# The chunk loop written out 27 times, or 6 times with a hardware loop of 7 trips between

## The chip, the cores and the metric

The kernel runs on one core of one Trainium2 chip. A NeuronCore has five engines that run their own instruction streams side by side and meet only at semaphores: TensorE (PE, matrix products), VectorE (DVE), ScalarE (ACT), GpSimd (POOL) and SyncE (SP, which here only issues transfers). The metric is the device time of one execution in microseconds (us), the median over several executions.

## The reference, cut to what matters

Three stages follow each other over 12480 tokens of 128 channels: an attention of 49 agents on the keys and of the queries on the agents, and then two two-layer networks of 2048 hidden units.

```
a2k = softmax(scale * agents @ k.T)            # 49 x 12480
agent_v = a2k @ v                              # 49 x 128
x = softmax(scale * q @ agents.T) @ agent_v    # 12480 x 128
h = x @ w_in                                   # 12480 x 2048
g = where(h >= 1, h, where(h <= -1, 0, (h + 1)**2 / 4))
x = g @ w_out                                  # 12480 x 128
r = maximum(x @ w_in2, 0)
out = (s * r*r + b) @ w_out2                   # 12480 x 128
```

## The kernel before, in words

The program is written engine by engine. Each engine has its list of instructions, and the order in it is the order of the source code; there is no scheduler. An instruction names the semaphore count that it waits for and the semaphore that it raises.

After a start-up part of some 55 us (keys and values, the agents' softmax, splitting the weights into a high and a low part in `fp32r` so that two or three products replace one in full precision), the tokens go through in 25 chunks of 500 (`W = 500`, the last chunk 480). A chunk has 16 *items* (`TILES = 16`), one for each block of 128 hidden units. For an item PE does 11 matmuls over 500 columns: 2 for the first network's hidden layer (`ps_h`, lines 559 and 560), 3 for the second network's hidden layer (`ps_h`, lines 578 to 580), 3 that add up the first network's output in `ps_y` (lines 541 to 543) and 3 that add up the second's in `ps_o` (lines 609 to 611). Between them the other engines work on the items: DVE makes `below` (L869), ACT squares it (L672), DVE adds it to `ps_h` (L882), ACT rounds the result to `g_hi` (L680), DVE forms the rest `g_lo` (L864), and PE may then use both for `ps_y`, two items later (`LAG1 = 2`). For the second network ACT takes the positive part (L701) and squares it (L710), and POOL splits it (L1015, L1016, L1018) for `ps_o`, again two items later. The second network is one chunk and four items behind the first. When a chunk's `ps_y` is complete, DVE copies it to `y` (L903, in item 1 of the next chunk), and only then may PE begin the next sum in the same bank (L541, in item 2).

These steps stand in a function `iteration(turns, phase)` of each engine. `all_iterations` calls it for i = 0 to 26, 25 chunks and two more in which the later steps of the last chunks are finished. The buffers form rings of 3 chunks, so the addresses in iteration i depend only on i mod 3 (`CHUNKS_PER_TRIP = 3`). Every semaphore count depends on i itself: item n waits, for instance, for `g1_split` to be at least n + 1. The helper functions accept i as a Python number or as a value in a register of the engine.

```
def at_least(eng, semaphore, count):
    if not isinstance(count, int) or count > 0:
        eng.wait_ge(semaphore, count)

i = turns * CHUNKS_PER_TRIP + phase
for j in range(TILES):
    n, place, there = item(i, phase, j, 0)
```

Before the change i is always a Python number, and the whole program is straight-line: 16412 instructions stand in the trace, 10314 of them PE's weight loads and matmuls.

Of the kernel before, what the change touches and what calls it, by code (L numbers as in the profile page):

```python
# [19 lines left out]
CHUNKS_PER_TRIP = 3  # L20
# [38 lines left out]
def build_program(nc, q, k, v, v_last, agents, w_in1, w_out1, w_in2, w_out2, s_b, out):  # L59
# [5 lines left out]
    CHUNKS = n_queries // W  # L65
# [5 lines left out]
    ITERATIONS = LAST_MLP2 // TILES + 1  # L71
# [4 lines left out]
    BLOCKS = KV_BLOCKS + 1  # L76
    KV_COLS = KV_TILES * 128

    assert C == 128 and n_queries == CHUNKS * W and n_agents < LOW
    assert n_tokens == KV_BLOCKS * KV_COLS + LAST_TILES * LAST_TOK  # L80
    assert MOD % H1_BANKS == 0 and MOD % H2_BANKS == 0 and MOD % SPLIT_RING == 0
# [2 lines left out]
    with ExitStack() as ctx:  # L84
# [232 lines left out]
                eng.wait_ge(semaphore, count)  # L317

        def all_iterations(eng, iteration):
            for i in range(ITERATIONS):  # L320
                iteration(*divmod(i, CHUNKS_PER_TRIP))


# [47 lines left out]
        def _(sp):  # L371
# [25 lines left out]
            def iteration(turns, phase):  # L397
# [7 lines left out]
                if there:  # L405
                    sp.wait_ge(out_ready, c + 1)
                    columns = width(c * TILES)
                    sp.dma_start(out[:, bass.ds(c * W, columns)], out_ring[:, slot, 0:columns]).then_inc(out_slot_free[slot], 16)

            all_iterations(sp, iteration)  # L410

            for slot in range(IO_RING):
# [4 lines left out]
        def _(pe):  # L417
# [128 lines left out]
            def iteration(turns, phase):  # L546
                i = turns * CHUNKS_PER_TRIP + phase
                for j in range(TILES):
# [49 lines left out]
                    if there:  # L598
# [13 lines left out]
                        mm.then_inc(g2_used, 1)  # L612

            all_iterations(pe, iteration)


        @block.scalar
        def _(act):
# [63 lines left out]
            def iteration(turns, phase):  # L682
                i = turns * CHUNKS_PER_TRIP + phase
                for j in range(TILES):
# [35 lines left out]
                    if j == MLP2_DELAY + LAG2 - 1 and chunk(i, phase, -2)[2]:  # L720
# [5 lines left out]
                        nc.scalar.activation(out_ring[:, slot, 0:columns], o_ps[:, 0:columns], ACT.Identity, bias=bias_col[:]).then_inc(out_ready, 1)  # L726

            all_iterations(act, iteration)


# [337 lines left out]
```

## Time and profile before

| | us |
|---|---|
| median of 3 runs | 1107.23 (1107.03 to 1107.34) |
| the profiled execution | 1107.03 |
| its span, first to last instruction | 1105.2 |
| PE busy in the span | 1091.7 |
| ACT / DVE / POOL busy | 923.7 / 915.3 / 841.6 |
| instruction packets fetched | 41 of 0.67 MB in all, 46 of 0.38 MB in all |

The time outside the span is 1107.03 - 1105.2 = 1.8 us. A row of the profile names an engine, a line of the code, the operation, `out<-in`, and its count. Matmuls overlap: a row's duration (0.39 us for 500 columns) is longer than the distance to the next one (0.23 us), and PE is counted busy as long as one of them runs. The queues called "instruction" are the transfers that bring the program itself from memory to the engines.

### The profile page before, as it was taken

What the parts mean: (1) busy time and instruction counts of PE and PEld (TensorE: products, weight loads), DVE (VectorE), ACT (ScalarE), POOL (GpSimd) and SP (SyncE); (2) the same over time, 40 slices, a digit from 0 to 9 for tenths busy, and PEclk for the clock granted to TensorE, in tenths of its full rate; (3) what the DMA queues carried; (4) which work ended last, traced back from release to release, by engine and by line L of the source; (5) the groups of instructions that cost most, each with busy time, mean ns of one, the idle gap of its engine ahead of it and who ended that gap; (6) DMA issues with size and microseconds to landing.
All of it is one profiled execution on the core that took longest, in us unless ns stands there. A gap on an engine that the chain in (4) does not pass through costs nothing.

```text
span 1105.2 us, 16412 instructions
## 1 busy us (share of the span) xinstructions
PE 1091.7 (99%) x5157; PEld 915.8 (83%) x5157; DVE 915.3 (83%) x1456; ACT 923.7 (84%) x1745; POOL 841.6 (76%) x1231
## 2 busy tenths in 40 slices
PE   9999999999999999999999999999999999999998
PEld 8867888888888888888888888888888888888886
DVE  4777888889888888888889888888888888888876
ACT  3276888888888888888888888888888888888887
POOL 3555888788788788788788788788788788788760
PEclk9998999999999999999999999999999999999999
DMA  9700000000000000000000000000000000000000
GB/s 367 287 1 1 1 19 20 1 20 19 1 20 19 1 19 20 1 20 19 1 19 20 1 20 19 1 19 19 3 18 19 10 11 19 13 7 10 10 1 19
DMA packets 11863, 30.84 MB, mean 28 GB/s; under 512 B 1568, under 2 KB 8192, under 8 KB 11264
## 3 DMA queue, kind: packets, MB, share of 16 engines
q1 hardware_dynamic: 11776, 29.79, 7.6%
q8 instruction: 41, 0.67, 0.3%
q14 instruction: 46, 0.38, 0.1%
HBM read 23.40 MB, written 6.39 MB: 27 GB/s over the span
## 4 chain that ended last, share of the span: by engine, by line
PE 97%; DVE 1%; ACT 1%; issue 0%; DMA 0%; SPq 0%; ACTq 0%; DVEq 0%
PE ps_y L541 8%; PE ps_h L559 8%; PE ps_h L578 8%; PE ps_h L580 8%; PE ps_o L609 8%; PE ps_h L579 8%; PE ps_h L560 8%; PE ps_y L542 8%; PE ps_o L610 8%; PE ps_y L543 8%; PE ps_o L611 8%; PE ps_h L446 2%; PE ps_job L424 2%; PE ps_o L472 1%; PE ps_y L472 1%; PE ps_job L432 1%
## 5 line engine op out<-in xcount | busy, mean ns | idle before, releaser
L1018 POOL TENSOR_TENSOR sb_g_lo<-sb_square,sb_g_hi 128x500 fp32r<-128x500 f32 x380 | 484.0, 1274 | 31.7
L882 DVE SCALAR_TENSOR_TENSOR ps_h<-sb_square,ps_h 128x500 f32<-128x500 f32 (+1 forms) x400 | 271.9, 680 | 119.4 <-ACT sb_square L672 118.4
L680 ACT ACTIVATE sb_g_hi<-ps_h 128x500 fp32r<-128x500 f32 (+1 forms) x400 | 235.1, 588 | 101.0 <-DVE ps_h L882 101.0
L864 DVE SCALAR_TENSOR_TENSOR sb_g_lo<-ps_h,sb_g_hi 128x500 fp32r<-128x500 f32 (+1 forms) x400 | 270.6, 677 | 20.2 <-ACT sb_g_hi L680 11.4
L869 DVE TENSOR_SCALAR sb_below<-ps_h 128x500 f32<-128x500 f32 (+1 forms) x380 | 256.7, 675 | 11.2 <-PE ps_h L560 9.9
L701 ACT ACTIVATE sb_relu<-ps_h 128x500 f32<-128x500 f32 (+1 forms) x400 | 235.3, 588 | 24.6 <-PE ps_h L580 11.3
L710 ACT ACTIVATE sb_square<-sb_relu 128x500 f32<-128x500 f32 (+1 forms) x400 | 245.6, 614 | 0.6
L672 ACT ACTIVATE sb_square<-sb_below 128x500 f32<-128x500 f32 (+1 forms) x380 | 233.7, 615 | 0.0
L1016 POOL TENSOR_SCALAR sb_g_hi<-sb_square 128x500 fp32r<-128x500 f32 x380 | 228.3, 601 | 0.0
L1015 POOL TENSOR_TENSOR sb_gate<-sb_ones 1x1 f32<-1x1 f32 x380 | 69.8, 184 | 152.2 <-ACT sb_square L710 150.8
L541 PE MATMUL ps_y<-sb_g_hi,sb_w_out_hi 128*128 128x500 f32 (+1 forms) x400 | 160.7, 402 | 1.2 <-DVE sb_g_lo L864 1.2
L559 PE MATMUL ps_h<-sb_probs_t,sb_m_hi 113*128 113x500 f32 (+1 forms) x400 | 159.3, 398 | 2.4 <-DVE sb_g_lo L864 2.2
L609 PE MATMUL ps_o<-sb_g_hi,sb_w_out_hi 128*128 128x500 f32 (+1 forms) x400 | 155.9, 390 | 1.4 <-DVE sb_g_lo L922 0.9
L578 PE MATMUL ps_h<-sb_y_hi,sb_w_in_hi 128*128 128x500 f32 (+1 forms) x400 | 156.0, 390 | 0.2 <-DVE sb_y_lo L908 0.2
L560 PE MATMUL ps_h<-sb_probs_t,sb_m_lo 113*128 113x500 f32 (+1 forms) x400 | 156.0, 390 | 0.0
L580 PE MATMUL ps_h<-sb_y_hi,sb_w_in_lo 128*128 128x500 f32 (+1 forms) x400 | 155.9, 390 | 0.0
L542 PE MATMUL ps_y<-sb_g_hi,sb_w_out_lo 128*128 128x500 f32 (+1 forms) x400 | 155.6, 389 | 0.0
L543 PE MATMUL ps_y<-sb_g_lo,sb_w_out_hi 128*128 128x500 f32 (+1 forms) x400 | 155.2, 388 | 0.0
L611 PE MATMUL ps_o<-sb_g_lo,sb_w_out_hi 128*128 128x500 f32 (+1 forms) x400 | 155.0, 387 | 0.0
L610 PE MATMUL ps_o<-sb_g_hi,sb_w_out_lo 128*128 128x500 f32 (+1 forms) x400 | 155.0, 387 | 0.0
L579 PE MATMUL ps_h<-sb_y_lo,sb_w_in_hi 128*128 128x500 f32 (+1 forms) x400 | 154.9, 387 | 0.0
L559 PEld LDWEIGHTS ps_h<-sb_probs_t,sb_m_hi 113*128 113x128 f32 x400 | 75.7, 189 | 19.7 <-DVE sb_g_lo L864 3.1
(109 smaller groups left out, 1266.7 us busy)
## 6 DMA issues: line engine op xcount, KB each, us to landing
sb_q_ring<-in_q SPq DMA_DIRECT2D x25, 250.0 KB, 2.8
sb_kv_ring<-in_k SPq DMA_DIRECT2D x12, 512.0 KB, 9.1
sb_kv_ring<-in_v SPq DMA_DIRECT2D x12, 512.0 KB, 15.7
out<-sb_out_ring SPq DMA_DIRECT2D x24, 250.0 KB, 2.1
sb_w_stage<-in_moe_w_out SPq DMA_DIRECT2D x2, 1024.0 KB, 11.7
sb_w_stage<-in_moe_w_in SPq DMA_DIRECT2D x1, 1024.0 KB, 17.8
sb_w_in<-in_moe_w_in SPq DMA_DIRECT2D x1, 1024.0 KB, 17.7
out<-sb_out_ring SPq DMA_DIRECT2D x1, 240.0 KB, 2.0
```

Of the source, the lines that this page charges most:

```text
L541: pe.matmul(y_ps[:, 0:width(n)], hi, g1_hi[:, slot, 0:width(n)], start=(f == 0), stop=False)
L542: pe.matmul(y_ps[:, 0:width(n)], lo, g1_hi[:, slot, 0:width(n)], start=False, stop=False)
L559: pe.matmul(h, m_hi[:, j * 128:(j + 1) * 128], probs_t[:, phase, 0:width(n)], start=True, stop=False)
L560: pe.matmul(h, m_lo[:, j * 128:(j + 1) * 128], probs_t[:, phase, 0:width(n)], start=False, stop=True).then_inc(h1_ready, 1)
L578: pe.matmul(h, hi, y_hi[:, y_slot, 0:width(n)], start=True, stop=False)
L580: pe.matmul(h, lo, y_hi[:, y_slot, 0:width(n)], start=False, stop=True).then_inc(h2_ready, 1)
L609: pe.matmul(o_ps[:, 0:width(n)], hi, g2_hi[:, slot, 0:width(n)], start=(f == 0), stop=False)
L710: nc.scalar.activation(square2[:, place2 % WORK_RING, 0:width(n2)], relu2[:, place2 % WORK_RING, 0:width(n2)], ACT.Square).then_inc(square ...
L864: nc.vector.scalar_tensor_tensor(g1_lo[:, slot, 0:columns], h1_bank(n, place), 0.0, as_f32(g1_hi[:, slot, 0:columns]), ALU.max, ALU.subtra ...
L869: nc.vector.tensor_scalar(below[:, place % WORK_RING, 0:width(n)], h1_bank(n, place), 1.0, 1.0, ALU.min, ALU.subtract).then_inc(below_read ...
L882: nc.vector.scalar_tensor_tensor(h, square1[:, place % WORK_RING, 0:width(n)], 1.0, h, ALU.min, ALU.add).then_inc(g1_summed, 1)
L1018: nc.gpsimd.tensor_tensor(g2_lo[:, place % SPLIT_RING, 0:columns], square, as_f32(hi), ALU.subtract).then_inc(g2_split, 1)
```

## The change

The 27 calls of `iteration` become 3 calls, a loop with `eng.Fori(0, TRIPS)` whose body holds 3 calls, and 3 calls behind it. With `CHUNKS = 25` it is `FIRST_FULL = 3`, `TRIPS = (25 - 1 - 3) // 3 = 7` and `END_FULL = 24`. So iterations 3 to 23 run in 7 trips, and each engine jumps back 6 times. In the loop `trip` is a register of the engine, so `turns`, `i` and all semaphore counts, and the token offset of the query load and of the output store, are computed by the engine itself.

```
-            for i in range(ITERATIONS):
+            for i in range(FIRST_FULL):
+                iteration(*divmod(i, CHUNKS_PER_TRIP))
+            with eng.Fori(0, TRIPS) as trip:
+                for n in range(CHUNKS_PER_TRIP):
+                    turns, phase = divmod(FIRST_FULL + n, CHUNKS_PER_TRIP)
+                    iteration(trip + turns, phase)
+            for i in range(END_FULL, ITERATIONS):
                 iteration(*divmod(i, CHUNKS_PER_TRIP))
```

The loop body of the built program, by engine (an instruction takes 64 bytes: 1.05 MB of fetched packets for 16412 instructions; on PE each of the 564 matmuls of a trip counts twice, with its weight load):

| engine | instructions in the body | KB | register operations in it |
|---|---|---|---|
| PE | 1239 | 79 | 98 + 6 |
| ACT | 408 | 26 | 119 + 5 |
| POOL | 257 | 16 | 62 + 3 |
| DVE | 227 | 15 | 56 + 1 |
| SP | 15 | 1 | 1 + 7 |

The first place is PE where the loop is entered, the first matmuls of iteration 3. In the names, `ps_h_0` is a bank of PSUM, and the names in brackets are the semaphores waited for. Before:

```order
L609 MATMUL ps_o<-sb_g_hi,sb_w_out_hi 128x500 [waits g2_split]
L610 MATMUL ps_o<-sb_g_hi,sb_w_out_lo 128x500
L611 MATMUL ps_o<-sb_g_lo,sb_w_out_hi 128x500
L559 MATMUL ps_h_0<-sb_probs_t,sb_m_hi 128x500 [waits g1_split,probs_t_ready]
L560 MATMUL ps_h_0<-sb_probs_t,sb_m_lo 128x500
L578 MATMUL ps_h_0<-sb_y_hi,sb_w_in_hi 128x500 [waits relu2_ready]
L579 MATMUL ps_h_0<-sb_y_lo,sb_w_in_hi 128x500
L580 MATMUL ps_h_0<-sb_y_hi,sb_w_in_lo 128x500
```

And the same place after the change, where line numbers are 9 higher:

```order
L618 MATMUL ps_o<-sb_g_hi,sb_w_out_hi 128x500 [waits g2_split]
L619 MATMUL ps_o<-sb_g_hi,sb_w_out_lo 128x500
L620 MATMUL ps_o<-sb_g_lo,sb_w_out_hi 128x500
L325 UNCONDITIONAL_BRANCH
L325 ISA
L320 ISA [waits probs_t_ready]
L568 MATMUL ps_h_0<-sb_probs_t,sb_m_hi 128x500 [waits g1_split]
L569 MATMUL ps_h_0<-sb_probs_t,sb_m_lo 128x500
L320 REGISTER_ALU
L587 MATMUL ps_h_0<-sb_y_hi,sb_w_in_hi 128x500 [waits relu2_ready]
L588 MATMUL ps_h_0<-sb_y_lo,sb_w_in_hi 128x500
L589 MATMUL ps_h_0<-sb_y_hi,sb_w_in_lo 128x500
```

The matmuls keep their order; register instructions (`REGISTER_ALU`, and `ISA`, several of them in one) stand between them, and some of these carry a wait that a matmul carried before.

The second place is the same one on ACT. Before:

```order
L672 ACTIVATE sb_square<-sb_below 128x500 [waits below_ready]
L710 ACTIVATE sb_square<-sb_relu 128x500 [waits g2_split,relu2_ready]
L680 ACTIVATE sb_g_hi<-ps_h_2 128x500 [waits g1_used,g1_summed]
L701 ACTIVATE sb_relu<-ps_h_0 128x500 [waits h2_ready]
L672 ACTIVATE sb_square<-sb_below 128x500 [waits below_ready]
L710 ACTIVATE sb_square<-sb_relu 128x500 [waits g2_split,relu2_ready]
```

After:

```order
L681 ACTIVATE sb_square<-sb_below 128x500 [waits below_ready]
L719 ACTIVATE sb_square<-sb_relu 128x500 [waits g2_split,relu2_ready]
L325 UNCONDITIONAL_BRANCH
L325 ISA
L320 REGISTER_ALU [waits g1_summed]
L689 ACTIVATE sb_g_hi<-ps_h_2 128x500 [waits g1_used]
L709 REGISTER_ALU
L710 ACTIVATE sb_relu<-ps_h_0 128x500 [waits h2_ready]
L679 REGISTER_ALU
L681 ACTIVATE sb_square<-sb_below 128x500 [waits below_ready]
```

Here up to three register operations come in for each item, and in 12 of the 48 items of a trip the wait for `g1_summed` stands on a register operation just ahead of the rounding.

The third place is the loop's end on ACT after the change, which the program before does not have:

```order
L681 ACTIVATE sb_square<-sb_below 128x500 [waits below_ready]
L719 ACTIVATE sb_square<-sb_relu 128x500 [waits g2_split,relu2_ready]
L325 REGISTER_ALU
L325 COMPARE_AND_BRANCH
L689 ACTIVATE sb_g_hi<-ps_h_2 128x500 [waits g1_used,g1_summed]
```

The branch follows the last square directly. If it is taken, what runs next is the `ISA` row at the start of the loop, some 400 instructions back.

## Rows read from the trace of the kernel before

**Rows 1.** The page: the span, the engines' busy time, the chain that ended last.

```profile
span 1105.2 us, 16412 instructions
...
PE 1091.7 (99%) x5157; PEld 915.8 (83%) x5157; DVE 915.3 (83%) x1456; ACT 923.7 (84%) x1745; POOL 841.6 (76%) x1231
...
PE 97%; DVE 1%; ACT 1%; issue 0%; DMA 0%; SPq 0%; ACTq 0%; DVEq 0%
```

**Rows 2.** Busy time by stretch (us, counts): the second and sixth trip's stretches.

```profile
289.60:413.10 123.50, 123.50 (x565) 103.41 (x565) 105.46 (x166) 108.31 (x205) 100.61 (x151) 1.00 0.04 13
...
783.50:907.00 123.50, 123.50 (x566) 103.39 (x565) 105.46 (x166) 108.29 (x205) 100.63 (x151) 1.00 0.05 14
```

**Rows 3.** Timeline of PE around 289.65: start, duration, operation.

```profile
288.97 0.39 PE L609 MATMUL ps_o<-sb_g_hi,sb_w_out_hi 128*128 128x500 f32 x1
...
289.65 0.39 PE L559 MATMUL ps_h<-sb_probs_t,sb_m_hi 113*128 113x500 f32 x1
...
293.74 0.39 PE L543 MATMUL ps_y<-sb_g_lo,sb_w_out_hi 128*128 128x500 f32 x1
...
295.78 0.38 PE L541 MATMUL ps_y<-sb_g_hi,sb_w_out_hi 128*128 128x500 f32 x1
```

**Rows 4.** Timeline of PE, the score matmuls of one chunk.

```profile
298.25 0.98 PE L424 MATMUL ps_job<-sb_agents_t,sb_q_ring 128*126 128x49 f32 x8
```

**Rows 5.** Who waited for whom, 289.6 to 413.1: total us, times, longest us.

```profile
POOL sb_gate L1015 <- ACT sb_square L710: 18.7, 39, 1.2
DVE ps_h L882 <- ACT sb_square L672: 15.3, 37, 0.6
ACT sb_g_hi L680 <- DVE ps_h L882: 12.6, 36, 1.1
```

**Rows 6.** DMA queues of the page: packets, MB, share of 16 engines' span.

```profile
q8 instruction: 41, 0.67, 0.3%
q14 instruction: 46, 0.38, 0.1%
```

**Rows 7.** DMA issues: KB each, median us to landing.

```profile
sb_q_ring<-in_q SPq DMA_DIRECT2D x25, 250.0 KB, 2.8
...
sb_agents_t<-in_agents SPq DMA_DIRECT2D x1, 24.5 KB, 1.8
```

**Rows 8.** Timeline of ACT around 289.65.

```profile
287.83 0.59 ACT L680 ACTIVATE sb_g_hi<-ps_h 128x500 fp32r<-128x500 f32 x1 [0.24 <-DVE ps_h L882]
288.48 0.59 ACT L701 ACTIVATE sb_relu<-ps_h 128x500 f32<-128x500 f32 x1
288.96 0.61 ACT L672 ACTIVATE sb_square<-sb_below 128x500 f32<-128x500 f32 x1
289.48 0.61 ACT L710 ACTIVATE sb_square<-sb_relu 128x500 f32<-128x500 f32 x1
290.33 0.59 ACT L680 ACTIVATE sb_g_hi<-ps_h 128x500 fp32r<-128x500 f32 x1 [0.24 <-DVE ps_h L882]
```

**Rows 9.** Timeline of DVE, the copy of a finished `ps_y`.

```profile
293.45 0.68 DVE L864 SCALAR_TENSOR_TENSOR sb_g_lo<-ps_h,sb_g_hi 128x500 fp32r<-128x500 f32 x1
294.17 0.68 DVE L903 COPY sb_y<-ps_y 128x500 f32<-128x500 f32 x1
```

**Rows 10.** Groups by line, 166.19 to 1030.45: shapes, count, busy us, mean ns.

```profile
L541 PEld LDWEIGHTS ps_y<-sb_g_hi,sb_w_out_hi 128*128 128x128 f32 x336 | 63.4, 189 | 10.9
```

**Rows 11.** Timeline of POOL, the split that frees L609 at 288.97.

```profile
286.02 1.29 POOL L1018 TENSOR_TENSOR sb_g_lo<-sb_square,sb_g_hi 128x500 fp32r<-128x500 f32 x1
```

**Rows 12.** Timeline of PE before 70 us, three rows with idle time ahead.

```profile
54.64 1.12 PE L510 MATMUL ps_h<-sb_w_in,sb_agent_v_t 128*113 128x128 f32 x4 [1.43 <-DVE sb_agent_v_t L850]
...
63.02 1.08 PE L424 MATMUL ps_job<-sb_agents_t,sb_q_ring 128*126 128x49 f32 x8 [0.95 <-DVE sb_m_lo L854]
...
69.22 0.49 PE L541 MATMUL ps_y<-sb_g_hi,sb_w_out_hi 128*128 128x500 f32 x1 [1.01 <-DVE sb_g_lo L864]
```

**Rows 13.** Busy time by stretch around them; the third last number is the clock.

```profile
50.00:55.70 5.70, 4.27 (x33) 3.53 (x32) 1.79 (x8) 0.27 (x1) 0.00 (x0) 1.00 0.00 1
55.70:59.10 3.40, 3.27 (x7) 1.92 (x7) 0.59 (x2) 1.46 (x3) 1.02 (x1) 0.50 0.00 0
...
62.00:67.00 5.00, 4.05 (x22) 3.28 (x22) 4.97 (x11) 3.14 (x6) 2.64 (x3) 1.00 0.00 0
67.00:72.00 5.00, 3.99 (x19) 3.09 (x19) 4.12 (x10) 4.66 (x9) 3.58 (x4) 1.00 0.02 5
```

More of the change, by code:

```diff
@@ L77, in build_program @@
     KV_COLS = KV_TILES * 128
+    FIRST_FULL = 3
+    TRIPS = (CHUNKS - 1 - FIRST_FULL) // CHUNKS_PER_TRIP
+    END_FULL = FIRST_FULL + TRIPS * CHUNKS_PER_TRIP
     assert C == 128 and n_queries == CHUNKS * W and n_agents < LOW
```

## The prediction, written before the changed kernel ran

> **What bounds the kernel now.** I read the page's busy line and chain first [rows 1]: PE is busy 1091.7 of 1105.2 us, and 97% of the chain that ended last is PE. The stretches of one trip's length come next [rows 2]: PE is busy 123.50 of 123.50 us, at a granted clock of 1.00, and ACT, DVE and POOL 108, 105 and 101. The 11 matmuls of an item follow each other at some 0.23 us, so an item takes 2.5 us, and nothing in these stretches ends a wait of PE. The waits of the others [rows 5] are ACT, DVE and POOL waiting for each other in PE's shadow. The change leaves every matmul and its order alone. So it can only gain where PE idles, and in the looped part PE never does: a gain is excluded there to within the measurement. It costs what it makes PE idle, and nothing else.
>
> **Part 1, register operations, steady state.** On PE they are 104 in 48 items, two an item. The trace has no such row. The nearest is the row of score matmuls [rows 4]: 8 matmuls and their 8 weight loads in 0.98 us, so PE's sequencer hands out an instruction in 0.06 us or less. An item's 22 then take 1.35 us and 2 more 0.12, of 2.5. I cost them at nothing; the cover is PE's array. From above, an operation as long as a whole hop between ACT and POOL, 18.7 / 48 = 0.39 us an item [rows 5], would come to 1.35 + 0.78 = 2.1, still under 2.5; below nothing it can't be, since it adds work. On ACT, DVE and POOL the operations stand mostly behind an instruction that is running (0.6 us or more), and none of them is on the path. In 12 of 48 items on ACT one stands in the hop from DVE's sum to ACT's rounding, where ACT idles 0.24 us [rows 8]. That hop belongs to a circle (square, sum, rounding, positive part, next square) which is only about 0.15 us short of PE's item time: L701 starts 0.65 after L680 at 287.83, and ACT can start one activation 0.50 after another, as 288.48, 288.96 and 289.48 show. One operation of up to 0.1 us fits in. SP's loads are issued a chunk (41 us) ahead of their use and land in 2.8 us [rows 7]. Cost: 0.
>
> **Part 2, the six jumps back.** The program is fetched in packets [rows 6]: 0.67 MB / 41 = 16 KB on PE's queue, 0.38 / 46 = 8 KB on the other's. 5157 matmuls with their weight loads are 10314 instructions of 64 bytes, 660 KB, in 41 such packets: each is fetched once, as the straight-line program reaches it. At the jump the loop's first packet may be gone. PE's body is 79 KB, 5 to 6 packets, ACT's 26 KB, 4 to 5, POOL's and DVE's 2 to 3. If it is gone, the engine stops for one fetch. No row shows one. From below: the smallest transfer lands in 1.8 us [rows 7], plus the packet's own time, 0.1% of 16 x 1105.2 us / 46 = 0.4 us for 8 KB: 2.2. With PE's packet, 0.3% of the same / 41 = 1.3 us: 3.1. From above: 2.8 + 1.3 = 4.1, the load of 250 KB with it. And zero, if the packet is still there. For ACT I take 2.7, midway between 2.2 and 3.1, as the 1.8 us is for a transfer issued with its addresses at hand.
>
> **What of it is hidden.** I take ACT, as its body is the longest of those with the small packets. Its sequencer gets to the branch when the last square has been let go, not before L701 has ended at 288.48 + 0.59 = 289.07 and not after 289.48, when that square starts [rows 8]. The next trip's first rounding starts at 290.33. That covers 1.26 to 0.85 us. What is late then passes along: the rounding's lateness shrinks by the 0.15 us of the circle, goes through square, sum and the next rounding to L864 at 293.45 and to the copy of `ps_y`, which runs right behind it [rows 9]. The copy ends at 294.17 + 0.68 = 294.85, and PE needs the bank at 295.78 [rows 3], with the weight load of 0.19 us before it [rows 10]: 0.74 us more. This is the tightest place; L541's other wait, for L864's result, ends 0.72 us before this one. Cover in all: 1.74 to 2.15, I take 1.9. PE idles 2.7 - 1.9 = 0.8 us in item 2 of a trip, six times: 4.8 us. POOL and DVE, if they miss too, stop in the same two us and add nothing to the chain: DVE's next sum would wait about as long as ACT's rounding.
>
> Sum: 1107.03 + 4.8 = 1111.8 us. The profiled execution (1107.03) is 0.2 below the median (1107.23), so I leave it there. Over the fetch's range, 2.2 to 4.1, it is 1108.8 to 1120.2.
>
> The Trainium skill ("Runtime: NRT & Kernel Launch", section on instruction fetch mechanics) says that a taken branch whose target isn't in the current two-page window forces a fetch, in blocks of 16 KiB, from an instruction memory of 32 KiB, or 128 KiB on PE. The trace agrees on the 16 KB of PE's packets and not on the others' 8 KB. By the window rule PE's head is gone too (the second rival); by the sizes PE's 79 KB and ACT's 26 KB fit, and nothing is gone (the first).
>
> **Rivals.**
> *Nothing is late* (not slower). Either the heads are all still held, or the fetch takes under 1.9 us and ends in the cover. For it: bodies of 79 and 26 KB are not large, and the fetch of 8 KB itself is 0.4 us. Against: each packet is fetched once now, so nothing shows that an old one is kept, and 1.8 us is a floor without any of the packet. It decides where the fetch is below 1.9 us. Time: 1107.2, within 0.2%.
> *PE's own head is gone.* PE's sequencer passes the last wait of a trip when POOL's split ends, 286.02 + 1.29 = 287.31 [rows 11]; its array has work until 289.65 [rows 3]. Less 0.4 us for six instructions to be handed out, that covers 1.9. Fetch 3.1: idle 1.2, six times 7.2: 1114.2; with 4.1, 1120.2. It overlaps with ACT's and doesn't add.
> The skill ("Advanced Engine Details and Errata", sequencer and instruction queues) gives PE a queue of 64 instructions in which they wait for their semaphores. By that its sequencer would be 64 x 2.5 / 22 = 7.3 us ahead, and a fetch on PE would cost nothing: 1111.8 or 1107.2, as ACT decides. No row shows how far it is ahead.
> *The clock falls with the stop.* PE idle for 1.43 us before 54.64 was followed by 3.4 us at 0.50, that is 1.2 GHz, while 0.95 and 1.01 us at 63 and 69 were not [rows 12, 13]. Between 1.0 and 1.4 us of idle it decides. Half speed for 3.4 us costs 1.7; with a fetch of 3.3 or more: 6 x (1.4 + 1.7) = 18.6, 1125.6.
> *Register waits are slower.* If a wait on a register's value ends 0.1 us later than one on a constant, the circle of ACT and DVE has two in each item: 0.20 - 0.15 = 0.05, times 336 items = 17 us, 1124. Below 0.075 each it costs nothing. Nothing in the trace speaks for it, and nothing excludes it.
>
> **How the numbers follow.** ACT's head late, 1111.8: 0.43. PE's too, 1114 to 1120: 0.15. Nothing late, 1107.2: 0.31. Clock or register waits, 1118 and more: 0.08. Faster, by something that I don't see: 0.03. What this measurement tells from no change is about 0.2%, 2.2 us. Of the first case a tenth stays below that (a fetch up to 2.3 us). So slower: 0.39 + 0.15 + 0.08 = 0.62; same 0.31 + 0.04 = 0.35; faster 0.03. The range goes from the case of nothing late, 1106.9, to 1119.5, which leaves out the clock and the longest fetches. The first case's own range is 1108.8 to 1115.
>
> **What would show it.** The span's stretches between jumps should be as long as before plus one short idle of PE, six times, ahead of the first matmul of `ps_y` (L550 now) in the third item of trips 2 to 7, put down to DVE's copy, with ACT idle some 2 us ahead of its rounding just before. If PE's head is gone, the idle stands at L568, the trip's first matmul, and waits for nothing shown. Some 6 to 12 packets would be fetched within a few us of the jumps. If matmuls in the middle of a trip are further apart than 0.23 us, or the idle is spread over all items, part 1 is wrong. I am wrong in the main if the time is below 1109.4 or if the idle is at the first matmul.

## The result

| | before | after |
|---|---|---|
| median, us | 1107.13 (1106.27 to 1109.47, 6 runs) | 1116.22 (1114.91 to 1118.35, 6 runs) |
| ratio | | 1.0079 (95%: 1.0065 to 1.0091) |
| the profiled execution, us | 1107.03 | 1118.42 |
| its span, us | 1105.2 | 1116.2 |
| first matmul of iteration 3 to first matmul of iteration 24, us | 864.26 | 872.44 |

The changed kernel is slower by 0.8%, 9.1 us. The forecast was 1111.8 with a range of 1106.9 to 1119.5: the sign and the engine that is late are right, the loss is twice what I forecast (4.6 over the median of before), and PE stands still at three places in a trip where I forecast one.

The page after the change, the lines that answer to [rows 1] and [rows 6]:

```profile
span 1116.2 us, 18675 instructions
...
PE 1099.4 (98%) x5157; PEld 916.8 (82%) x5157; DVE 912.2 (82%) x1456; ACT 918.1 (82%) x1745; POOL 844.0 (76%) x1231
...
q14 instruction: 51, 0.42, 0.1%
q8 instruction: 14, 0.23, 0.1%
...
PE 89%; issue 3%; ACT 3%; DVE 3%; DMA 0%; ACTq 0%; SPq 0%; DVEq 0%
```

Of PE's packets 14 are left of 41: the loop's body is fetched once and stays, the *head* too, the packet in which the body begins. On the other queue 51 packets came, more than the 46 of the straight-line program, though the engines on it now have far less code: there something is fetched again and again. The chain that ended last runs over ACT, DVE and "issue" for 9% of the span, where it was 97% PE.

Where the time went is seen by stretches, as in [rows 2] (us, each engine's busy time and counts, clock third from the end). The first stretch lies inside the first trip. The second begins just before 292.55, PE's first matmul behind the first jump, and holds one chunk, the third holds two, the fourth is the next jump's chunk:

```profile
169.00:292.50 123.50, 123.50 (x566) 103.36 (x565) 105.30 (x165) 107.76 (x206) 100.94 (x151) 1.00 0.05 14
292.50:335.10 42.60, 41.96 (x189) 34.20 (x189) 34.73 (x55) 35.52 (x69) 33.59 (x51) 1.00 0.04 13
335.10:417.40 82.30, 82.30 (x377) 68.87 (x377) 70.19 (x110) 71.84 (x137) 67.27 (x101) 1.00 0.04 13
417.40:460.00 42.60, 42.05 (x190) 34.27 (x190) 34.79 (x56) 35.62 (x69) 33.66 (x51) 1.00 0.04 13
```

Inside a trip PE is busy all the time, as before; in the chunk behind a jump it idles 0.6 us, and the slots around the idle pieces are stretched too. Measured from first matmul to first matmul of a chunk, the six chunks behind a jump take 42.44 to 42.59 us, all others 41.15 or 41.16. The six differences add up to the 8.18 us of the table: 1.36 us a jump.

The two profiled executions differ by 11.4 us. Of the other 3.2 us, 0.4 lie outside the span (2.2 us there against 1.8), and 2.9 in the start-up part, with the same instructions ahead of iteration 3 in both. It ended at 166.19 us in one and 169.08 in the other; over the thirteen profiled executions of this study it ends anywhere from 163.50 to 169.08 us, in whichever kernel, the changed one alone at 169.08 and 167.88.

PE's pace shows where this comes from. Two stretches of the start-up part, first 5 to 9 us before and after the change, then the one behind the 1.43 us of idle of [rows 12], after the change and in a later run (four trips):

```profile
5.00:9.00 4.00, 3.88 (x35) 3.91 (x36) 0.74 (x1) 2.12 (x5) 0.00 (x0) 1.00 1.03 417
5.00:9.00 4.00, 3.90 (x18) 3.93 (x19) 0.00 (x0) 1.76 (x3) 0.00 (x0) 1.00 1.03 420
...
58.90:62.30 3.40, 3.40 (x7) 1.69 (x6) 1.19 (x2) 1.68 (x3) 1.02 (x1) 0.50 0.00 0
55.70:59.10 3.40, 3.27 (x12) 1.93 (x11) 1.34 (x3) 2.59 (x5) 1.36 (x2) 1.00 0.00 0
```

In the first pair PE did 35 matmuls in one execution and 18 in the other, busy in both: it went at half the pace. The trace's first record of the granted clock, at 1.00, begins at 4.5 us before and at 11.1 after (the view shows 1.00 ahead of that record too). Over the thirteen, where it begins at 4.4 to 6.3 us iteration 0 starts at 55.5 to 56.1, and where it begins at 9.3 to 11.1 us, at 57.7 to 58.5. Then the clock falls to 0.50, the 1.2 GHz level, for 3.4 us near 57 us in seven of the thirteen, and for 6.8 us near 92 in seven (six have both): iterations 0 to 2 take 107.6 us without a fall, 110.0 to 110.6 with both. All this varies between executions of one program: the timed runs of the kernel before have a mean granted clock of 0.995 in some and of 0.999 or 1.000 in others. I therefore compare kernels by the stretch from iteration 3 to iteration 24 ("the looped part", 864.26 us before), beside the medians of the timed runs.

Now the first jump itself. What line 325, the loop, put on the engines' sequencers between 289 and 296 us (duration in ns as min/median/max, then first and last start in us):

```profile
L325 PEldq COMPARE_BRANCH  x1: 251/251/251, 290.4 to 290.4; - x1
L325 PEldq FUSED_REGOPS  x1: 59/59/59, 290.7 to 290.7; - x1
L325 DVEq COMPARE_BRANCH  x1: 63/63/63, 291.4 to 291.4; - x1
L325 DVEq FUSED_REGOPS  x1: 67/67/67, 291.8 to 291.8; - x1
...
L325 ACTq COMPARE_BRANCH  x1: 45/45/45, 292.1 to 292.1; - x1
...
L325 POOLq COMPARE_BRANCH  x1: 45/45/45, 293.9 to 293.9; - x1
L325 POOLq FUSED_REGOPS  x1: 68/68/68, 294.2 to 294.2; - x1
L325 ACTq FUSED_REGOPS  x1: 59/59/59, 295.0 to 295.0; - x1
```

On PE, DVE and POOL the first instruction of the next trip stands 0.3 to 0.4 us behind the branch. On ACT it stands 2.9 us behind. In the other five jumps ACT's stop is 2.82, 2.75, 2.90, 2.80 and 2.81 us; the mean of the six is 2.83. The register operations are short: the median of one is 32 to 40 ns by engine, and several in one (`FUSED_REGOPS`) take 37 to 77.

ACT's timeline there answers to [rows 8]:

```profile
291.37 0.59 ACT L710 ACTIVATE sb_relu<-ps_h 128x500 f32<-128x500 f32 x1
291.86 0.61 ACT L681 ACTIVATE sb_square<-sb_below 128x500 f32<-128x500 f32 x1
292.37 0.61 ACT L719 ACTIVATE sb_square<-sb_relu 128x500 f32<-128x500 f32 x1
295.16 0.59 ACT L689 ACTIVATE sb_g_hi<-ps_h 128x500 fp32r<-128x500 f32 x1 [2.17 <-PE ps_y L552]
```

In the undisturbed rhythm the rounding (L689) starts 0.85 us after the last square, at 293.22. It is 1.94 us late. The releaser named in the bracket is misleading: the view puts an idle stretch down to the last semaphore that it finds, and the sequencer's rows above show what it was waiting for, its next instruction. PE and DVE stand still for ACT soon after. DVE and PE behind the jump, the rows that answer to [rows 9] and [rows 3]:

```profile
295.78 0.68 DVE L873 SCALAR_TENSOR_TENSOR sb_g_lo<-ps_h,sb_g_hi 128x500 fp32r<-128x500 f32 x1 [1.90 <-ACT sb_g_hi L689]
...
298.78 0.67 DVE L912 COPY sb_y<-ps_y 128x500 f32<-128x500 f32 x1
...
303.85 1.19 DVE L917 TENSOR_TENSOR sb_y_lo<-sb_y,sb_y_hi 128x500 fp32r<-128x500 f32 x1
```

```profile
292.55 0.39 PE L568 MATMUL ps_h<-sb_probs_t,sb_m_hi 113*128 113x500 f32 x1
...
296.51 0.49 PE L550 MATMUL ps_y<-sb_g_hi,sb_w_out_hi 128*128 128x500 f32 x1 [0.17 <-DVE sb_g_lo L873]
...
299.58 0.49 PE L550 MATMUL ps_y<-sb_g_hi,sb_w_out_hi 128*128 128x500 f32 x1 [0.31 <-DVE sb_y L912]
...
305.17 0.49 PE L587 MATMUL ps_h<-sb_y_hi,sb_w_in_hi 128*128 128x500 f32 x1 [0.17 <-DVE sb_y_lo L917]
```

PE is stopped at three places, not one: at L550 in item 1 (for the `g_lo` of the trip's last item), at L550 in item 2 (for the copy of `ps_y`, the one that I had forecast), and at L587 in item 4 (for `y_lo`, the low part of the copied `y`, which the second network needs from item 4 on). The distances between the first matmuls of items 0 to 5 are 2.50, 2.93, 3.06, 3.35, 2.91 us, where before they are 2.50, 2.50, 2.48, 3.36, 2.46: 0.43, 0.58 and 0.45 us more. A wait of 0.17 to 0.31 us in the row costs more than that, since the weight load behind it is late too and the matmul takes 0.49 instead of 0.39.

The view of who waited for whom, over 160 to 1040 us, shows that it is the same behind the jumps (total us, times, longest; the wait for `y_lo` is long enough to be listed in five of the six), as against [rows 5], where PE did not stand:

```profile
ACT sb_g_hi L689 <- DVE ps_h L891: 92.5, 242, 1.2
DVE sb_g_lo L873 <- ACT sb_g_hi L689: 23.5, 73, 1.9
ACT sb_g_hi L689 <- PE ps_y L552: 14.5, 12, 2.2
...
PEld ps_y L550 <- DVE sb_g_lo L873: 7.4, 12, 0.7
...
PE ps_y L550 <- DVE sb_y L912: 1.9, 6, 0.3
PE ps_h L587 <- DVE sb_y_lo L917: 0.8, 5, 0.2
```

### The profile page after: what moved, and what is told of

Its sections match the earlier page's. It is cut to its first block, busy times and chain, and to the rows that moved or that the text cites. A ratio compares the mean times of both kernels' runs of the same rounds, so it can differ in the third digit from the quotient of the medians.

```text
span 1116.2 us, 18675 instructions
## 1 busy us (share of the span) xinstructions
PE 1099.4 (98%) x5157; PEld 916.8 (82%) x5157; DVE 912.2 (82%) x1456; ACT 918.1 (82%) x1745; POOL 844.0 (76%) x1231
## 4 chain that ended last, share of the span: by engine, by line
PE 89%; issue 3%; ACT 3%; DVE 3%; DMA 0%; ACTq 0%; SPq 0%; DVEq 0%
PE ps_h L587 8%; PE ps_y L550 8%; PE ps_h L589 8%; PE ps_h L568 8%; PE ps_h L588 8%; PE ps_o L618 7%; PE ps_h L569 7%; PE ps_y L551 7%; PE ps_y L552 7%; PE ps_o L619 7%; PE ps_o L620 7%; PE ps_h L455 2%; PE ps_job L433 1%; PE ps_o L481 1%; ACT sb_g_hi L689 1%
## 5 line engine op out<-in xcount | busy, mean ns | idle before, releaser
L689 ACT ACTIVATE sb_g_hi<-ps_h 128x500 fp32r<-128x500 f32 (+1 forms) x400 | 235.8, 590 | 119.3 <-DVE ps_h L891 104.8
L878 DVE TENSOR_SCALAR sb_below<-ps_h 128x500 f32<-128x500 f32 (+1 forms) x380 | 256.5, 675 | 11.1 <-PE ps_h L569 10.3
L550 PE MATMUL ps_y<-sb_g_hi,sb_w_out_hi 128*128 128x500 f32 (+1 forms) x400 | 162.1, 405 | 3.6 <-DVE sb_y L912 1.9
L587 PE MATMUL ps_h<-sb_y_hi,sb_w_in_hi 128*128 128x500 f32 (+1 forms) x400 | 156.6, 391 | 1.1 <-DVE sb_y_lo L917 1.0
L550 PEld LDWEIGHTS ps_y<-sb_g_hi,sb_w_out_hi 128*128 128x128 f32 x400 | 75.6, 189 | 22.3 <-DVE sb_g_lo L873 9.9
```

The source lines that it names most:

```text
L550: pe.matmul(y_ps[:, 0:width(n)], hi, g1_hi[:, slot, 0:width(n)], start=(f == 0), stop=False)
L587: pe.matmul(h, hi, y_hi[:, y_slot, 0:width(n)], start=True, stop=False)
L689: nc.scalar.activation(g1_hi[:, place % SPLIT_RING, 0:width(n)], h1_bank(n, place), ACT.Relu).then_inc(g1_hi_ready, 1)
L878: nc.vector.tensor_scalar(below[:, place % WORK_RING, 0:width(n)], h1_bank(n, place), 1.0, 1.0, ALU.min, ALU.subtract).then_inc(below_read ...
```

## The experiments

All were made from the changed kernel. The theory was: the whole loss is ACT's stop at the jumps, while its packet of instructions is fetched, and what of it gets past the slack of the chain to PE. The rivals were that the loop costs something on another engine, that the register operations cost, and that the slower kernel is an accident of the start-up part. This table has what each run gave; "stop" is the time from ACT's branch to the first instruction of the next trip, the looped part is 864.26 us before. Where ACT's body begins at a set slot, ACT also stops once on entering the loop, for 2.4 to 2.7 us, and the looped part holds that too: 1.1 us at slot 0, 1.2 at 92, 0.7 for both shorter bodies and 1.3 for hint and slot 0. The six jumps alone are 6.0, 6.2, 0, 5.0 and 0 us there.

| | median, us | ratio (95%) | looped part | stop | packets, PE's / others' queue |
|---|---|---|---|---|---|
| changed | 1116.22 | 1.0079 (1.0065-1.0091) | +8.18 | 2.75-2.91 | 14 / 51 |
| ACT alone loops | 1114.43 | 1.0062 (1.0042-1.0082) | +7.6 | 2.70-3.12 | 41 / 69 |
| all but ACT loop | 1107.47 | 0.9996 (0.9980-1.0012) | +0.0 | none | 14 / 28 |
| ACT's head at slot 0 | 1114.23 | 1.0066 (1.0043-1.0089) | +7.2 | 2.40-2.69 | 14 / 46 |
| ACT's head at slot 92 | 1115.64 | 1.0069 (1.0045-1.0092) | +7.5 | 2.40-2.69 | 14 / 47 |
| ACT with a prefetch hint | 1111.23 | 1.0031 (1.0017-1.0044) | +2.9 | 1.82-2.01 | 14 / 46 |
| shorter body, slot 0 | 1109.99 | 1.0014 (1.0002-1.0026) | +0.7 | 0.23-0.26 | 14 / 15 |
| shorter body, slot 92 | 1113.49 | 1.0055 (1.0035-1.0075) | +5.7 | 2.41-2.67 | 14 / 46 |
| six chunks a trip | 1111.19 | 1.0029 (1.0009-1.0049) | +3.6 | 2.69-2.74 | 46 / 69 |
| hint and slot 0 | 1112.93 | 1.0051 (1.0035-1.0067) | +1.3 | 0.20-0.23 | 14 / 16 |
| four trips | 1111.08 | 1.0035 (1.0021-1.0048) | +3.98 | 2.78-2.83 | 28 / 50 |
| changed, once more | 1115.82 | 1.0072 (1.0049-1.0095) | +7.86 | 2.73-2.97 | 14 / 51 |

The kernel before, timed beside them, had medians between 1107.2 and 1109.1, in single runs 1104.2 to 1110.0.

### ACT alone in the loop, and all engines but ACT

Each engine builds its own loop, so one can jump while the others run their code written out. In the first kernel:

```
         def all_iterations(eng, iteration):
+            if eng.engine != mybir.EngineType.Activation:
+                for i in range(ITERATIONS):
+                    iteration(*divmod(i, CHUNKS_PER_TRIP))
+                return
```

and in the second `==` stands for `!=`. Expected of the first:

> Only ACT runs iterations 3 to 23 in the loop; PE, DVE, POOL and SP are straight-line as before. Theory A (ACT stands still 2.9 us at each of its six jumps because the first packet of its loop is no longer held, and PE loses 1.2 to 1.5 us each time): 1107.1 + 8 = 1115, the same idle of PE in items 2 to 5 of trips 2 to 7. Theory B (the loss comes from register operations and register waits on PE, DVE and POOL, or from their jumps): 1107 to 1109.

Expected of the second:

> ACT is straight-line; the other four engines run the loop. Theory A: 1107.1 within 1 us, no idle of PE in the looped part, although PE, DVE, POOL and SP jump six times and do all their register operations. Theory B: 1113 to 1116.

ACT alone brings 7.6 of the 8.18 us, the four others together bring none: their looped part is equal to before to the hundredth of a microsecond. The waits of both kernels over 170 to 1027 us, first ACT alone:

```profile
ACT sb_g_hi L693 <- DVE ps_h L895: 89.3, 235, 1.1
DVE sb_g_lo L877 <- ACT sb_g_hi L693: 24.1, 75, 2.1
ACT sb_g_hi L693 <- PE ps_y L556: 14.9, 12, 2.4
...
PE ps_y L554 <- DVE sb_y L916: 1.4, 6, 0.2
```

And all but ACT, where PE has no row:

```profile
ACT sb_g_hi L693 <- DVE ps_h L895: 90.3, 250, 1.2
DVE sb_below L882 <- PE ps_h L573: 8.6, 21, 0.4
...
DVE sb_g_lo L877 <- ACT sb_g_hi L693: 5.5, 28, 0.2
```

In this second kernel PE, DVE and POOL execute all their register operations, and wait on register values, in every item. So these cost nothing in time, as part 1 of the prediction said. ACT's own register waits are in the changed kernel, whose chunks away from the jumps take the same 41.15 us as before, so the rival of slower register waits falls. A jump whose packet is there costs nothing either.

### Half the jumps

```
-            with eng.Fori(0, TRIPS) as trip:
+            with eng.Fori(0, 4) as trip:
 ...
-            for i in range(END_FULL, ITERATIONS):
+            for i in range(15, ITERATIONS):
```

> The loop runs 4 trips (iterations 3 to 14) and the other 9 iterations are written out: 3 jumps instead of 6, all else as in the changed kernel. Theory A: half the loss, looped part and what follows together 4.1 us longer than before, time 1111. If the loss came with the loop as such (entering and leaving it, or its register operations in each trip): between 1111 and 1115, not in the ratio of the jumps 3 to 6 but of the trips 4 to 7 or as a constant.

Three jumps brought 3.98 us, 1.33 each, with stops of 2.8 us as before. The price goes with the number of jumps, and the chunks that are longer are those behind them.

### Where the head of ACT's loop stands in its packet

An option of the loop sets the slot within a packet at which its first instruction stands:

```
-            with eng.Fori(0, TRIPS) as trip:
+            slots = {eng.engine: 0} if eng.engine == mybir.EngineType.Activation else None
+            with nc.Fori(0, TRIPS, engines=OrderedEngineSet([eng.engine]), head_slot=slots) as trip:
```

The second kernel has 92 for 0.

> All five engines loop as in the changed kernel; the only edit is where ACT's body lies in the program: its first instruction stands at the start of a fetched packet, so the 408 instructions end 24 into the fourth packet of 128, and the packet behind is not yet asked for at the jump. Theory A with four packets of 8 KB held: the head is still there, the jump costs ACT 0.3 us as it does on DVE and POOL, 1107.1 to 1108. Rival A2 (no packet behind the current and the next is ever kept): ACT stops as before, 1115.

> The same, with ACT's body starting 92 instructions into a packet, so that it ends at 500, 116 into the fourth packet: still four packets, but the fifth is asked for about 50 instructions (15 us) ahead of the jump. Theory A with a fifth packet pushing out the first: ACT stops, but the fetch is alone in its queue: 2.2 to 2.9 us at each jump, 1110 to 1115. If four packets are kept whatever is fetched ahead: 1107.

With slot 0 I had counted on the head being still held. It wasn't: the stops only went from 2.83 us to between 2.40 and 2.69, and both placements fetch 5 packets a trip. ACT's body has 408 instructions, 3.2 packets of 128, so it touches 4 even at slot 0; a fifth, the one behind the body, is fetched ahead. I had counted on that not being asked for yet; at slot 0 its transfer stands at 407.58, 6.6 us ahead of ACT's second jump at 414.16, about where ACT enters the fourth. Either the number held is 4 and that one pushes the head out, or nothing that was executed is ever held. The next pair decides it.

### A shorter body at two placements

Two waits on ACT that, as I read the program, others imply are left out inside the loop (they are kept in the straight-line parts). This takes 93 instructions out of the body and leaves 315:

```
-                    at_least(act, g1_used, n - SPLIT_RING + 1)
+                    if isinstance(n, int):
+                        at_least(act, g1_used, n - SPLIT_RING + 1)
 ...
-                        at_least(act, g2_split, n2 - WORK_RING + 1)
+                        if isinstance(n2, int):
+                            at_least(act, g2_split, n2 - WORK_RING + 1)
```

At slot 0 it touches 3 packets, at slot 92 it touches 4.

> As the changed kernel, but in the loop ACT leaves out two waits that other waits already imply (for g2_split before the second square, for g1_used before the rounding), so its body has 315 instructions instead of 408, and it starts at the start of a packet of 128. It touches 3 packets, and the one fetched ahead makes 4. Theory A with 4 packets of 8 KB held: no refetch, a gap of 0.3 us at the jump, 1107 to 1108. Rival A2 (only the current packet and the next are held): 2.9 us at each jump, 1113 to 1115.

> The same instructions as the run before, with ACT's body starting 92 instructions into a packet: it ends at 407, touches 4 packets, and with the one ahead 5. Theory A with 4 packets held: ACT refetches all of them in each trip and stops some 2.3 to 2.9 us at each jump, 1112 to 1115, although the body is no longer than in the run before. If the length alone decides (315 against 408): as the run before, 1107 to 1108.

The same instructions, moved by 92 places, cost 0.23 to 0.26 us or 2.41 to 2.67 us at each jump. The first jump at slot 0:

```profile
L327 ACTq COMPARE_BRANCH  x1: 50/50/50, 292.7 to 292.7; - x1
L327 ACTq FUSED_REGOPS  x1: 59/59/59, 292.9 to 292.9; - x1
```

and at slot 92:

```profile
L327 ACTq COMPARE_BRANCH  x1: 50/50/50, 290.3 to 290.3; - x1
...
L327 ACTq FUSED_REGOPS  x1: 59/59/59, 292.7 to 292.7; - x1
```

At slot 0 the chunks behind the jumps take 41.15 us like all others, and from the second trip on no packet is fetched inside the loop: 15 on the queue against 46. What is left of the loss, 0.7 us, comes once, when ACT enters the loop. So a packet that was executed is held, and what decides is the packets that the body touches, plus one ahead: 4 (shorter body, slot 0) fit, 5 (shorter body at slot 92, full body at slot 0 and 92) don't. This pair also shows that the stop is a fetch and not the price of a jump. On ACT the rule is tested at 4 and at 5 packets; of PE, DVE and POOL the runs show only one body that fits and one that doesn't.

### Asking for the packet ahead of the jump

```
+            with nc.Fori(0, TRIPS, engines=OrderedEngineSet([eng.engine]), hint_back_edge=eng.engine == mybir.EngineType.Activation) as trip:
```

> As the changed kernel, with one more instruction at the start of ACT's loop body that names the jump to come, so that the packet asked for ahead of the jump is the loop's first and not the one behind the loop. Theory A (ACT's first packet is no longer held at the jump, and fetching it is the whole stop): the gap from ACT's branch to its next register operation falls from 2.9 to 0.3 us and the time to 1107 to 1108.5. Rival C (a taken jump on a body this long costs its time whatever is held): 1115.

It missed what I expected of it. The hint, one instruction at the body's head, names the jump to come, but what it brought was not early enough: the stop went down to 1.82 to 2.01 us, not to 0.3. In the trace of the changed kernel two packets are fetched at the second jump, 0.35 and 1.16 us after ACT's branch at 416.98, the first of them the useless one behind the loop; with the hint it is one, 0.35 us after the branch. The time is instructive all the same. The looped part is 2.9 us longer than before, 0.48 a jump, for a stop of 1.9; PE has next to no waits at the first two places, and at the first jump only the third is left:

```profile
299.66 0.39 PE L569 MATMUL ps_h<-sb_probs_t,sb_m_hi 113*128 113x500 f32 x1
300.42 0.49 PE L588 MATMUL ps_h<-sb_y_hi,sb_w_in_hi 128*128 128x500 f32 x1 [0.15 <-DVE sb_y_lo L918]
```

So `y_lo`, and not the copy of `ps_y`, is the tightest place.

Then the hint together with slot 0:

> Hint and placement together on ACT, with the body of 409 instructions: it starts at the start of a packet, so the jump stands 25 instructions into the fourth packet, and the packet named by the hint can be asked for some 7 us ahead of the jump. In the run with the hint alone the jump stood 5 instructions into the fifth packet, the named packet was asked for 0.8 us ahead, and the stop was still 1.9 us. Theory A (the stop is the fetch of the head, less what of it is done before the jump): gap at the jump 0.3 us, the looped part 864.3 us as before, time 1107 to 1108. Rival (the hint itself helps by about 1 us and no more): gap 1.5 us or more, looped part 866 or more.

At the jumps the stop is gone, 0.20 to 0.23 us, with all chunks at 41.15, though the body has its 408 instructions: the four packets that it touches fit, since what is asked for at the end of the body is the head and no fifth packet. The time did not: 1112.93. In the profile, 1.3 us are what a stop of 2.7 us on entering the loop costs, and the part behind iteration 24 is 1.6 us longer (76.4 against 74.8 us). With the hint alone that part is 0.9 us longer, in the ten kernels without a hint it is not (74.7 to 74.8); I put it down to the packet behind the loop, which the hint keeps from being fetched ahead, but no run isolates that. The profiled execution is 6.0 us over that of before: 1.3 and 1.6, 0.4 outside the span, and 2.8 in a start-up part that ended at 168.94 us, with the late rise and both falls of the clock. The five timed executions lie at 1112.4 to 1113.1, so they seem to have had the same start-up; it is not the change's.

### A body too large for PE

```
-            with eng.Fori(0, TRIPS) as trip:
-                for n in range(CHUNKS_PER_TRIP):
+            with eng.Fori(0, 6, 2) as trip:
+                for n in range(2 * CHUNKS_PER_TRIP):
 ...
-            for i in range(END_FULL, ITERATIONS):
+            for i in range(21, ITERATIONS):
```

> The loop's body holds 6 chunks instead of 3 (iterations 3 to 20 in 3 trips, so 2 jumps). PE's body is then some 2470 instructions, 158 KB, about 10 packets of 16 KB, ACT's 816, and DVE's and POOL's over 450. Theory A with 128 KB held on PE: PE's own head is now gone too, its stop shows as a gap of about 3 us behind its branch and some 1 to 2 us of idle at the trip's first matmul; with the delays through ACT 2 x 1.4 to 2.5: 1110 to 1112. If PE holds more than that, only ACT's delays remain: 1110.

PE's body is now 2478 instructions, 155 KB, and its head is gone at both jumps; 46 packets are fetched on its queue where 14 were. DVE and POOL miss too. What PE's timeline then looks like at the first jump:

```profile
412.67 0.39 PE L620 MATMUL ps_o<-sb_g_lo,sb_w_out_hi 128*128 128x500 f32 x1
414.78 0.49 PE L568 MATMUL ps_h<-sb_probs_t,sb_m_hi 113*128 113x500 f32 x1 [1.72 <-issue]
```

This is the rival of the prediction in which PE's own head is gone, in a kernel where it is true: one idle stretch at the trip's first matmul, released by nothing ("issue"). PE's stops are 3.87 and 3.34 us, its idle 1.72 and 1.19 us, the loss 2.0 and 1.6 us (43.04 + 41.25 and 42.50 + 41.40 us for the two chunks behind each, against 2 x 41.15). ACT's stop of 2.7 us goes on beside it; what the loss exceeds PE's idle by is 0.3 and 0.4 us, and ACT's part can be no more than that. The total, 3.6 us for two jumps, is less than the changed kernel's 8.18 for six, because there are fewer jumps, while each costs more. The granted clock stayed at 1.00 behind 1.72 us of idle.

### The changed kernel once more

> The changed kernel once more beside the kernel before on one chip. The looped part 8.2 us longer as in its first profile, since the jumps cost the same each time; the part ahead of the loop need not repeat the 2.9 us that it was longer there, as the two programs are the same instructions up to the loop. Time 1114 to 1117.

1115.82 us and a looped part 7.86 us longer: the loss is no accident of one execution.

## Why the prediction was right, and what it under-estimated

**Part 1, register operations, 0.** Right. 41.15 us a chunk with and without them, and 0.9996 for the kernel in which four engines have them.

**Whose head is gone.** Right for ACT. PE's head is held, as the first half of the rival "nothing is late" assumed for all engines. I had no row that told PE from ACT; that it was ACT and not PE, or neither, was a guess at 0.43 that came true. Not only the head is gone: ACT's packets are all fetched anew in each trip, six a trip with the useless one, three of them within 3.5 us of the jump (I had expected 6 to 12 in all). Only the head's fetch stops ACT. POOL and DVE do not miss; I had left that open and it changed nothing. By the window rule of the Trainium skill ("Runtime: NRT & Kernel Launch", Instruction fetch mechanics) PE's head would be gone as well; the runs contradict that, since PE and the shorter ACT body at slot 0 jump back over 5 to 6 and 3 packets in 0.2 to 0.35 us. By the sizes on the same page of the Trainium skill, 32 KiB or 128 KiB on PE, four packets of 8 KB or eight of 16 KB fit: that agrees with every run here, once the packet fetched ahead is counted.

**The stop, 2.7 us.** Measured 2.83. It is inside the bounds of 2.2 to 4.1. Part of it is the useless packet, fetched first, which I had not thought of: where that one comes earlier (slot 0 and 92) the mean is 2.5. That my 2.7 lies so close is in part luck.

**The cover to the rounding, 0.85 to 1.26 us.** Measured 2.91 - 1.94 = 0.97 at the first jump. Right.

**The circle's 0.15 and the copy's 0.74.** From the trip's first matmul to the copy it was 294.17 - 289.65 = 4.52 us before and is 298.78 - 292.55 = 6.23 now, 1.71 late: 0.23 were won back. The copy's slack is 0.80 if PE starts 0.13 us behind its end, as it does at 299.58. So by item 2 PE has lost 1.71 - 0.80 = 0.9 us; measured are 0.43 + 0.58 = 1.01. For this place the working was right, 0.8 forecast. That a first part of it falls in item 1 already, on `g_lo`, does not add.

**"This is the tightest place".** This is the step that failed. Behind the copy I had looked no further. `y_lo` ends at 303.85 + 1.19 - 292.55 = 12.49 us into the trip. In the trace of before, `y_lo` and PE's first matmul of that item's three stand at

```profile
299.20 1.08 DVE L908 TENSOR_TENSOR sb_y_lo<-sb_y,sb_y_hi 128x500 fp32r<-128x500 f32 x1
...
300.94 0.39 PE L578 MATMUL ps_h<-sb_y_hi,sb_w_in_hi 128*128 128x500 f32 x1
```

DVE's row gives 299.20 + 1.08 - 289.65 = 10.63, so `y_lo` is 1.86 us late, with next to nothing of the rounding's 1.94 won back. The slack of `y_lo` is 300.94 - 0.13 - 300.28 = 0.53 us, where 300.28 is the end of `y_lo` and 0.13 the time from that to PE's start, against 0.80 for the copy. So PE loses 1.86 - 0.53 = 1.33 us in all by item 4; measured are 1.44 at this jump and 1.36 in the mean. Cover in all is 2.83 - 1.36 = 1.5 us and not 1.9. The sum with the numbers measured: 6 x (2.83 - 0.97 - 0.53) = 8.0, against 8.18 in the trace. With a stop of 1.9 us the same formula gives 0.4 a jump, and the kernel with the hint lost 0.48; with ACT's head at slots 0 and 92 (mean stop 2.49 and 2.52) it gives 1.0, and these lost 1.00 and 1.04. It is 0.1 to 0.2 too high for ACT alone in the loop (2.90, lost 1.27) and for the shorter body at slot 92 (2.54, lost 0.83).

**8.18 or 9.1.** The medians differ by 9.1 us, the looped parts by 8.2 (7.9 in the repetition). Of the last 0.9 us, 0.4 stand outside the span: 2.1 to 2.2 us in every execution of the changed kernel, 1.7 to 1.9 in every one of before; what they are no run shows (1.8 where ACT alone loops). The other 0.5 us is within what the start-up part varies between executions (5.6 us from the earliest to the latest). The latest of each kernel, 1118.4 and 1110.0, are 8.4 apart.

**The rivals.** Nothing is late: fell, as the stops are 2.75 us and more. PE's own head gone: not in this kernel, shown to be real with twice the body, where the fetch took 3.3 to 3.9 us (3.1 forecast) and 2.15 of it were covered (1.9 forecast). The clock falls: fell, PE's idle pieces are 0.31 us or less, and even 1.72 us at once didn't lower it in a busy stretch, while 1.43 us ahead of 54.64 had been followed by a lower clock [rows 12, 13]. The bound between 1.0 and 1.4 us was wrong: the same idle of 1.43 to 1.44 us stands in the start-up part of all thirteen profiled executions, and the clock fell behind it in seven and stayed at 1.00 in six. Idle length alone does not decide it. Slower register waits: fell.

No version beat the kernel before. The two that come next to it in the looped part (all but ACT in the loop, equal, and the shorter ACT body at slot 0, 0.7 us behind) have nothing to gain there, since PE is busy for every microsecond of it.

## What to carry to other kernels

Before you roll up a long straight-line kernel, count for each engine the packets that the body touches, from its first slot to its last, plus one, and compare with what that engine holds; on ACT here 92 slots in where the loop begins decided between 0.2 us and 2.4 to 2.7 us a jump. If the head isn't held, leave that one engine's code written out, rather than all engines' (nothing lost here), or make fewer jumps (three instead of six halved the loss); longer trips help too, but once PE's own body no longer fits a jump costs 1.8 instead of 1.36 us. When you follow a lateness to the engine that bounds the kernel, don't stop at the first place that gives way: follow each product of the late chain to its last reader, and take the one with the least slack.

## What the runs showed of the hardware

- The packets of ACT's instructions are 8 KB, 128 instructions, and four are held, the one fetched ahead among them (a body that touches three stays, one that touches four only with the hint); of PE's 16 KB packets a body of 79 KB is held and one of 155 KB is not.
- A jump back whose head is held takes 0.20 to 0.35 us on the sequencer. One whose head is gone takes 2.4 to 3.1 us on ACT with 8 KB (2.7 to 3.5 on DVE and POOL with six chunks a trip), and 3.3 to 3.9 us on PE with 16 KB.
- A register operation takes 32 to 40 ns on the sequencer (medians by engine), several in one instruction 37 to 77 ns, a branch 38 to 67 ns, on PE 215 to 251 where it is taken and its head is held.
- PE's branch stands at 290.36, its array reaches the trip's first matmul at 292.55: its sequencer is 2.2 us ahead, some 19 instructions at 22 in 2.5 us. That is what a fetch on PE can hide in; with stops of 3.87 and 3.34 us it idled 1.72 and 1.19 us, 2.15 us less each time. The queue of 64 instructions of the Trainium skill ("Advanced Engine Details and Errata", sequencer and instruction queues) would have hidden both; no run here shows it that deep.
- An identical start-up part takes between 163.5 and 169.1 us in different executions. Some 2 to 3 us of it go with the first record of the granted clock (4.4 to 6.3 or 9.3 to 11.1 us), and 2.5 to 3.0 with two falls to 0.50, of 3.4 and 6.8 us, that come in some executions and not in others behind the same idle of PE. In all that is more than half of the differences studied here, so a comparison of single executions must be made on a stretch that leaves it out.
